# A fused gated linear attention and two MLPs: both steps of a level in one half slot, and the MLP's element work ahead of the attention's in each slot

## The reference, cut to what matters

```python
# B, H, S, D = 4, 8, 768, 48; everything float32
f = 1 / (1 + np.exp(-f_logit))
for t in range(S):                      # gated linear attention
    state = f[:, :, t, :, None] * state + einsum('bhd,bhe->bhde', k[:, :, t], v[:, :, t])
    y[:, :, t] = einsum('bhd,bhde->bhe', q[:, :, t], state)
x = y as [3072 tokens, 384]
h = x @ w_in                            # first MLP, d_ff 2048
g = where(h >= 1, h, where(h <= -1, 0, (h + 1) ** 2 / 4))
x = g @ w_out
z = x @ w_gate                          # second MLP, d_ff 1536
out = (z * sigmoid(z) * (x @ w_val)) @ w_out2
```

## Time and profile before

| | |
|---|---|
| median of 3 runs | 1079.31 us (1077.73 to 1080.3) |
| profiled execution, device time | 1078.47 us |
| its span in the trace | 1076.7 us |
| PE busy | 1015.5 us (94%) |
| DVE, ACT, POOL busy | 547.0, 445.2, 450.8 us |
| mean granted TensorE clock | 0.979 |

### The profile page before, as it was taken

The page is one execution under the profiler, slowest core; times in us unless marked ns, Lnnn a source line. Parts: engine busy times, 40 slices in busy tenths (PEclk is TensorE's granted clock), DMA queues, the critical chain, the costliest instruction groups (busy, mean ns, idle before and its releaser), DMA issues.

```text
span 1076.7 us, 19206 instructions
## 1 busy us (share of the span) xinstructions
PE 1015.5 (94%) x7816; PEld 828.8 (77%) x7816; DVE 547.0 (51%) x745; ACT 445.2 (41%) x808; POOL 450.8 (42%) x368
## 2 busy tenths in 40 slices
PE   2477899999999999999999999999999999999997
PEld 2465677778778777877788888888888888888886
DVE  7965965884686488568736532223222222222221
ACT  3439538544753855375336532122222222222221
POOL 3956962763564476447327422121221212212121
PEclk9569999999999999999999999999999999999999
DMA  9423005003300600220043110010010010000000
GB/s 357 158 72 145 1 2 216 31 2 124 122 1 2 216 30 2 82 107 2 2 177 131 45 39 22 1 59 1 1 59 1 1 59 1 30 1 1 30 1 29
DMA packets 17367, 63.52 MB, mean 59 GB/s; under 512 B 1920, under 2 KB 2176, under 8 KB 16512
## 3 DMA queue, kind: packets, MB, share of 16 engines
q1 hardware_dynamic: 17280, 62.30, 15.8%
HBM read 52.85 MB, written 9.44 MB: 58 GB/s over the span
## 4 chain that ended last, share of the span: by engine, by line
PE 83%; issue 5%; DVE 5%; ACT 3%; POOL 3%; DMA 1%; SPq 0%; POOLq 0%; ACTq 0%; DVEq 0%
PE acc L445 10%; PE acc L447 10%; PE acc L446 10%; PE bank L473 7%; PE bank L471 7%; PE bank L472 7%; PE hid L431 6%; PE bank L344 5%; PE hid L432 5%; PE hid L433 5%; DVE scores L748 3%; PE hid L473 2%; PE hid L472 2%; PE hid L471 2%; PE bank L376 2%
## 5 line engine op out<-in xcount | busy, mean ns | idle before, releaser
L939 POOL TENSOR_TENSOR g_lo<-prod,g_hi 128x512 fp32r<-128x512 f32 x72 | 93.1, 1293 | 347.4 <-ACT g_hi L650 347.4
L932 POOL TENSOR_TENSOR g_lo<-act_tmp,g_hi 128x512 fp32r<-128x512 f32 x96 | 140.5, 1463 | 188.8 <-ACT g_hi L611 188.8
L837 DVE TENSOR_TENSOR sig<-sig,bank 128x512 f32<-128x512 f32 x72 | 49.6, 688 | 275.9 <-ACT sig L644 275.9
L748 DVE COPY_PREDICATED scores<-mask,bank 64x512 f32<-64x512 int32 x144 | 134.2, 932 | 28.4 <-PE bank L344 26.6
L650 ACT CAST g_hi<-prod 128x512 fp32r<-128x512 f32 x72 | 44.9, 624 | 247.6 <-PE acc L447 247.6
L892 POOL TENSOR_TENSOR keys<-keys,gates 128x512 f32<-128x512 f32 x82 | 110.2, 1343 | 44.1 <-PE bank L344 32.7
L611 ACT CAST g_hi<-act_tmp 128x512 fp32r<-128x512 f32 x96 | 59.6, 621 | 164.1 <-DVE act_tmp L825 164.1
L344 PEld LDWEIGHTS bank<-right_q,keys 128*64 128x64 f32 x2304 | 81.0, 150 | 58.8 <-issue 54.6
L344 PE MATMUL bank<-right_q,keys 128*64 128x64 f32 x2304 | 91.0, 238 | 36.0 <-ACT right_q L546 28.1
L445 PE MATMUL acc<-g_hi,wout_hi 128*128 128x512 f32 x288 | 117.0, 406 | 8.0 <-POOL g_lo L932 8.0
L431 PE MATMUL hid<-x_hi,win_hi 128*128 128x512 f32 x288 | 119.0, 413 | 4.0 <-DVE act_tmp L825 4.0
(11 more groups left out here) (80 smaller groups left out, 1851.6 us busy)
## 6 DMA issues: line engine op xcount, KB each, us to landing
gates<-in_f_dram SPq DMA_DIRECT2D x12, 512.0 KB, 5.3
queries<-in_q_dram SPq DMA_DIRECT2D x12, 512.0 KB, 5.4
keys<-in_k_dram SPq DMA_DIRECT2D x12, 512.0 KB, 4.7
values<-in_v_tok_dram SPq DMA_DIRECT2D x6, 1024.0 KB, 8.8
q_tok<-in_q_tok_dram SPq DMA_DIRECT2D x12, 384.0 KB, 8.6
k_tok<-in_k_tok_dram SPq DMA_DIRECT2D x12, 384.0 KB, 9.0
x_dram<-x_out SPq DMA_DIRECT2D x6, 768.0 KB, 3.9
x_raw<-x_dram SPq DMA_DIRECT2D x6, 768.0 KB, 5.5
```

The source lines that it names most:

```text
L748: last = dve.copy_predicated(o, level_mask(li, half), t[rows(half), :].rearrange("p (x b r) -> p x b r", x=BP, r=m))
L932: pool.tensor_tensor(g_lo[:, c % RING, :], act_tmp[:, 2 + c % 2, :], g_hi[:, c % RING, :].bitcast(F32), ALU.subtract).then_inc(g_lo_done, 1)
```

## The change

Three things are changed, and no instruction is added or removed.

1. The plans' `step` tables: steps 2i and 2i+1 of a level, which had half slots of their own, share one.
2. On ACT `square(m, c)` is issued in slot c, between the two attention calls, and no longer at the start of slot c+1; `split_g1` of chunk c-1 takes its place at the start of the slot.
3. On DVE `activate` and `clamp`, and on POOL `split_g1`, are issued ahead of the slot's first attention call.

```diff
 USUAL = Plan(own=(-9, -8), diag=(-8, -7), place=(-6, -5, -4, -3), sigmoid=(-2, -1), gated=(-1, 0),
-             step=(1, 3, 5, 7, 8, 9, 10, 12, 13, 14, 15, 17, 18, 19), last_merge=21,
+             step=(1, 1, 4, 4, 7, 7, 10, 10, 13, 13, 15, 15, 18, 18), last_merge=21,
 SECOND = Plan(own=(-9, -8), diag=(-8, -7), place=(0, 2, 3, 4), sigmoid=(3, 4), gated=(4, 5),
-              step=(6, 8, 9, 10, 11, 12, 13, 14, 16, 17, 18, 19, 20, 21), last_merge=22,
+              step=(6, 6, 9, 9, 12, 12, 14, 14, 16, 16, 18, 18, 20, 20), last_merge=22,
...
@@ ACT, loop over m and c
                 if m > 0 or c > 0:
-                    square(*((m, c - 1) if c else (m - 1, FC1 - 1)))
+                    split_g1(*((m, c - 1) if c else (m - 1, FC1 - 1)))
                 for a, place in turns(m, 2 * c):
                     attention(a, place)
-                if m > 0 or c > 0:
-                    split_g1(*((m, c - 1) if c else (m - 1, FC1 - 1)))
+                square(m, c)
                 for a, place in turns(m, 2 * c + 1):
                     attention(a, place)
...
@@ ACT, before the second MLP
-                    square(UNITS - 1, FC1 - 1)
                     split_g1(UNITS - 1, FC1 - 1)
...
@@ DVE, loop over m and c
-                for a, place in turns(m, 2 * c):
-                    attention(a, place)
                 if m > 0 or c > 0:
                     activate(*((m, c - 1) if c else (m - 1, FC1 - 1)))
                 clamp(m, c)
+                for a, place in turns(m, 2 * c):
+                    attention(a, place)
                 for a, place in turns(m, 2 * c + 1):
                     attention(a, place)
...
@@ POOL, loop over m and c
+                if m > 0 or c > 0:
+                    split_g1(*((m, c - 1) if c else (m - 1, FC1 - 1)))
                 for a, place in turns(m, 2 * c):
                     attention(a, place)
-                if m > 0 or c > 0:
-                    split_g1(*((m, c - 1) if c else (m - 1, FC1 - 1)))
                 for a, place in turns(m, 2 * c + 1):
                     attention(a, place)
```

## The result

| | before | after |
|---|---|---|
| median | 1079.12 us (4 runs) | 1103.34 us (1102.74 to 1104.01, 4 runs) |
| ratio | | 1.0225 (95% interval 1.0207 to 1.0243) |
| span of the profiled execution | 1076.7 us | 1100.9 us |
| mean granted TensorE clock | 0.979 | 0.973 |

The account below looks back on a forecast made before the run. PE was taken as the bound from MLP units 1 to 4, DVE and POOL before. -5.9 + 19.2 + 4.4 - 2.0 + 0 + 3.4 = +19.1 gave 1097.6, with 0.8 to the median 1098 us; range 1081 to 1110.

Parts of the forecast that it names:

- Part 1: PE, two steps back to back in MLP units 1 to 4: a pair saves 0.21 us, -5.9 us in all.
- Part 2: Slot 3 of units 1 to 4: PE waits 4.3 to 5.2 us at step 4 for ACT's copies, +19.2 us.
- The releaser's name: Sign in the profile after: PE's waits on ACT's right_q grow by some 16 to 20 us.
- Part 3: Unit boundary, slots 13 to 15: ACT idles for the clamp, chunk 14's low part late; +1.1 a unit, +4.4 us.
- Part 4: Lead-in: keys of step 11 now ahead of POOL's token products, so PE's wait of 4.82 goes; -2.0 us.
- by the sum of DVE's operations: Lead-in: the outputs, which start at 67.37, can start some 2 us earlier, when step 12 has been read.
- Part 5: MLP unit 0 beside unit 1's state pass: DVE and POOL full with the same sum; 0, bounds -3 and +5 us.
- Part 6: TensorE's clock: each stall at step 4 may bring 3.4 us of half clock, costing 1.7; middle of 0 to 6.8, +3.4 us.
- Behind it nothing else is late: After the wait at step 4: steps 6 and 7 come a slot and a half later, with readings of 1.47 us.

Follow-up runs that it names:

- e3: The changed kernel with ACT's old order put back (square of the chunk before, copies, cast): 1082.38 us.
- e7: The changed kernel with ACT's cast of the chunk before moved behind the first attention call's copies, in slots 0 to 9 only: 1079.39 us.
- e5: The changed kernel with DVE reading only the first half of steps 0 to 3 in units 2 to 5, all orders kept: 1075.60 us.
- e10: The changed kernel with POOL's old order put back (keys and merges of the slot's first half ahead of the low part): 1093.76 us.
- e6: The changed kernel with DVE reading only the first half of steps 2 and 3 in units 2 to 5: 1088.11 us.
- e12: The kernel before with the usual plan's diagonal blocks one half slot earlier, both sigmoids in half slot -2, both gatings in -1: 1079.84 us.

## Why the prediction was right, point by point

- **Part 1, the pairs: right in kind, too small.** Forecast 0.21 a pair. By the count of the forecast, a pair takes 423.27 to 425.94 = 2.67 us less two pitches of 0.23 = 2.21, where two single steps take 2 x 1.27: 0.33 less. The 64 small matmuls fill 2.01 us (423.59 to 425.60), where I had 2 x 1.09 = 2.18: part of the 1.09 of a single step is the change of shape too. The sum over unit 3 agrees. Without its waits it is 96.05 - 1.57 = 94.48 before, and 102.36 - 6.46 (slot 3 over 6.32) - 3.22 (boundary) - 0.58 (slot 6) = 92.10 after: 2.4 us for seven pairs, 0.34 a pair. The pair in the timeline of PE of the kernel after:

```profile
423.27 0.39 PE L433 MATMUL hid<-x_hi,win_lo 128*128 128x512 f32 x1
423.59 2.08 PE L344 MATMUL bank<-right_q,keys 128*64 128x64 f32 x64
425.60 0.50 PE L445 MATMUL acc<-g_hi,wout_hi 128*128 128x512 f32 x1
425.94 0.39 PE L446 MATMUL acc<-g_lo,wout_hi 128*128 128x512 f32 x1
```

- **Part 2, the wait at step 4: right in mechanism, place and size.** Forecast 4.3 to 5.2 us in each unit's slot 3, measured 5.10, at 19.87 behind the hidden block (19.1 to 20.1). Each link is in the rows of after shown above; e3 and e7 cut the link cast to copies, e5 shortens the readings, and both remove it. The scalings' hold by POOL was at its upper end (the pair took 2.38 and not 1.4; e10: 1.1 us). The Trainium skill, "SBUF — State Buffer", section Who interferes with whom, says that a VectorE instruction with two SBUF inputs contends with a GpSimd one that reads SBUF; the trace agrees. The Trainium skill, "TensorEngine Tiling (Array Packing)", section PSUM Bottleneck, warns that tiling does not speed up the emptying of PSUM; the trace agrees here too, as halving the readings of four steps took 27.7 us off. The forecast's own terms end at 20.0, not 20.1, a slip without effect. The releaser's name was forecast wrongly: the profile has "issue" and not ACT's right_q.
- **Part 3, the boundary: right.** Forecast +1.1 a unit. In unit 3 slots 15 and 0 lose 0.08 + 3.14 = 3.22 us after (slot 0 over 6.32), and 0.79 + 0.78 = 1.57 before: +1.6. Over units 1 to 4 it is 0.1, 1.6, 1.6 and 2.3, together 5.7 where 4.4 were forecast. The cause holds too: ACT idles for 1.96 us for the clamp (1.8 to 2.2 forecast), the cast of chunk 14 came 1.4 behind the start of slot 0, its low part was late by 1.15, and the copies stood behind it (timelines of ACT and PE of the kernel after):

```profile
375.07 0.64 ACT L604 ACTIVATE act_tmp<-act_tmp 128x512 f32<-128x512 f32 x1 [1.96 <-DVE act_tmp L816]
...
385.80 0.61 ACT L611 CAST g_hi<-act_tmp 128x512 fp32r<-128x512 f32 x1
...
387.90 0.47 PE L445 MATMUL acc<-g_hi,wout_hi 128*128 128x512 f32 x1 [1.15 <-POOL g_lo L930]
391.41 1.15 PE L344 MATMUL bank<-right_q,keys 128*64 128x64 f32 x32 [1.20 <-issue]
```

  What I missed is small: in slot 0 of the changed kernel, too, the copies stand behind a cast (that of chunk 15), e7's edit took 0.2 of it.
- **Part 4, the lead-in: wrong, 0 instead of -2.** The keys of step 11 are indeed ahead of the token products, and PE no longer waits 4.82 for them as in the earlier trace rows. But the outputs start at 67.33 as before. The step that failed is "by the sum of DVE's operations": I took DVE's operations at their undisturbed length and as if they followed each other. POOL's token products, which now stand behind the keys of step 11 too, held DVE's two reductions by 0.22 + 0.81, and the two scalings behind them, beside POOL's keys, took 2.87 instead of 1.4: together the 2 us and a little more. POOL is busy for 13.24 of the 13.40 us from 54.0 to 67.4 in either kernel (timelines of DVE, POOL and PE of the kernel after):

```profile
58.03 3.59 POOL L877 TENSOR_TENSOR q_tok<-q_tok,k_tok 128x768 f32<-128x768 f32 x2
61.66 0.95 DVE L708 TENSOR_REDUCE diag<-q_tok 128x16 f32<-128x768 f32 x1 [0.81 <-POOL q_tok L877]
62.52 2.87 DVE L729 TENSOR_TENSOR queries<-queries,gates 128x512 f32<-128x512 f32 x2
63.34 2.97 POOL L890 TENSOR_TENSOR keys<-keys,gates 128x512 f32<-128x512 f32 x2
65.42 3.65 DVE L753 COPY scores<-bank 64x128 f32<-64x128 f32 x16
...
67.33 1.51 PE L376 MATMUL bank<-scores,values 128*32 128x128 f32 x24 [7.45 <-DVE scores L753]
```

- **Part 5, MLP unit 0: right.** Unit 1 starts at 181.44 against 181.26. The first step of unit 1 started at 96.91 (97.5 forecast), behind a gap of 5.53. The hidden block of chunk 3 starts 4.2 us later than before (103.78 against 99.59), and by unit 1 this is made up; by what, beyond the saved edges, no run tells apart.
- **Part 6, the clock: right in kind.** It fell in all four units, not in the two that the middle stood for, but each fall costs 1.0 to 1.2 us (e6), not 1.7: 4.0 to 4.8 where 3.4 were put. The 1.7 was half of 3.4, as if PE ran full for all of it. Part of the stretch is the small matmuls of steps 4 and 5, and those of step 5 wait for their copy anyway: at a granted clock of 1.00 the two groups take 2.35 us behind a wait (502.97 to 505.32 in e6) and 2.01 without. That is 0.34 of the missing 0.5 to 0.7; the rest is open.
- **Slot 6: missed.** It takes 6.77, and 6.19 in e7, where the cast stands behind the copies: 0.58 a unit. The step that failed is "Behind it nothing else is late". It is the same chain once more, at steps 8 and 9: their copies stand behind the cast of chunk 5, which waits for the maximum behind the readings of steps 6 and 7 (timelines of ACT and PE of the kernel after):

```profile
430.31 0.62 ACT L611 CAST g_hi<-act_tmp 128x512 fp32r<-128x512 f32 x1 [5.20 <-DVE act_tmp L823]
430.84 2.52 ACT L546 COPY right_q<-queries 64x512 f32<-64x512 f32 x4
...
432.18 2.42 PE L344 MATMUL bank<-right_q,keys 128*64 128x64 f32 x64 [0.17 <-issue]
```

The sum was 5 us too low. To it add, over the whole kernel: the lead-in's and unit 0's 2.2, the boundary's 1.3, slot 6's 2.3, the clock's 1.0, and 2.1 for the wait at step 4 (5.3 a unit in slot 3 without the clock, against 4.8); take off the 3.6 by which the pairs are better. That the total came within 5 us is in part luck: errors of 9 us one way met one of 4 us the other way.

## What to carry to other kernels

When two pieces of work that one engine consumes are put together, follow every list in which something stands behind them, and from each to the next engine: here four readings on DVE were covered everywhere except where ACT's copies stood behind a cast that needs DVE's next instruction. Putting an instruction first because it is always needed early is only free where what it waits for is ready; in the slots with readings the cast did better behind the copies (e7), and in the slots with diagonal blocks ACT's changed order did better than the old one (e3 against e7, 2.9 us a unit). And where PE waits for "issue" with a weight load in front, the releaser is found by reading the other engines' lists backwards from the moment at which PE goes on.

## What the runs showed of the hardware

- A stretch of half clock (3.4 us) came behind some waits of 2.1 us and not behind others of the same length (2.06 and 2.10 with, 2.04 and 2.08 without, in e6). It cost 1.0 to 1.2 us of time where PE was the bound, and nothing in e10, where it fell into work ahead of another wait (slot 3 is 10.57 us with it and 10.57 to 10.58 without).
- In the lead-in a full clock brought nothing. In e12 it was 1.00 from 21 to 66 us, where it was 0.61 in the earlier trace rows, and the first hidden block started later (78.7 us against 77.6), since DVE and POOL are the bound there (e12's windows):

```profile
21.00:66.00 45.00, 25.57 (x384) 23.14 (x384) 42.57 (x46) 21.73 (x33) 41.22 (x35) 1.00 0.38 148
```

- A group of 32 small matmuls between large ones took 1.27 us of PE's time, two groups back to back 2.21 and not 2.54: the changes of shape that a pair saves are worth 0.33 us.
- Reading 64x512 values out of PSUM under a mask took DVE 1.33 to 1.36 us each in steps 0 to 3, and 0.70 to 0.76 from step 4 on, with the same number of elements. What differs is the length of the runs in which they are written (1 or 2 elements, then 4 and more); that this is the reason was not tested.
